# A chunk's scores on six levels of two sub-blocks instead of three levels of four, and unit 1's transposed keys copied by VectorE

## The reference

```python
for t in range(S):
    state = alpha[:, :, t, :, None] * state + np.einsum('bhd,bhe->bhde', k[:, :, t], v[:, :, t])
    y[:, :, t] = np.einsum('bhd,bhde->bhe', q[:, :, t], state)
x = y.transpose(0, 2, 1, 3).reshape(B * S, H * D)

p = domain_probs / (domain_probs.sum(-1, keepdims=True) + 1e-09)
for e in range(E):
    out += p[:, e:e + 1] * (np.maximum(x @ w1[e], 0.0) @ w2[e])

h = out @ w_in
result = (h - np.tanh(h)) @ w_out
```

## Time and profile before

| | us |
|---|---|
| median of 3 runs (lowest, highest) | 1383.19 (1381.79, 1383.29) |
| the profiled execution | 1381.91 |
| its span | 1380.1 |
| TensorE busy (share of the span) | 1338.2 (97%) |
| VectorE busy | 874.3 (63%) |
| ScalarE busy | 573.4 (42%) |
| GpSimd busy | 277.2 (20%) |
| mean granted clock of TensorE | 0.989 of full |

### The profile page before, as it was taken

How to read it: one execution, slowest core, us unless ns; L and a number is a source line. 1 busy time by engine, 2 the same in 40 slices (tenths; PEclk the granted TensorE clock), 3 DMA queues, 4 the chain that set the end, 5 groups by cost and what they waited for, 6 DMA issues and landing times.

```text
span 1380.1 us, 25841 instructions
## 1 busy us (share of the span) xinstructions
PE 1338.2 (97%) x10177; PEld 1121.9 (81%) x10177; DVE 874.3 (63%) x1767; ACT 573.4 (42%) x1072; POOL 277.2 (20%) x274
## 2 busy tenths in 40 slices
PE   3699999999999999999999999999999999999999
PEld 3578788988878888878898887888887889888888
DVE  8984855994654875465687565497556378323285
ACT  1525346843214751414662323374231476211175
POOL 4666654004022001313001403100221000000000
PEclk8799999999999999999999999999999999999999
DMA  7389797856655656565655655664665465655552
GB/s 217 92 306 321 240 323 242 322 212 219 211 196 197 231 181 218 181 211 196 242 183 179 222 194 199 207 229 169 216 211 172 161 220 189 222 185 200 180 193 89
DMA packets 104680, 289.08 MB, mean 209 GB/s; under 512 B 9936, under 2 KB 64432, under 8 KB 104560
## 3 DMA queue, kind: packets, MB, share of 16 engines
q1 hardware_dynamic: 104416, 287.23, 60.9%
q10 hardware_dynamic: 144, 0.20, 0.1%
HBM read 242.52 MB, written 42.52 MB: 207 GB/s over the span
## 4 chain that ended last, share of the span: by engine, by line
PE 89%; DVE 7%; ACT 2%; issue 1%; DMA 0%; DVEq 0%
PE bank L662 14%; PE bank L663 13%; PE bank L664 13%; PE bank L687 9%; PE bank L688 9%; PE bank L689 9%; PE bank L713 4%; PE bank L711 4%; PE bank L712 4%; PE bank L575 4%; PE bank L616 2%; PE bank L553 1%; DVE RG L1166 1%; PE bank L588 1%; DVE GG L1136 1%
## 5 line engine op out<-in xcount | busy, mean ns | idle before, releaser
L887 ACT ACTIVATE HH<-GG 128x512 fp32r<-128x512 f32 x192 | 121.2, 631 | 631.4 <-PE bank L689 509.2
L662 PE MATMUL bank<-XB,RG 128*128 128x512 f32 x864 | 348.5, 403 | 4.7 <-DVE GG L1109 2.2
L663 PE MATMUL bank<-XB,RG 128*128 128x512 f32 x864 | 339.4, 393 | 0.0
L664 PE MATMUL bank<-XB,RG 128*128 128x512 f32 x864 | 338.3, 392 | 0.0
L1109 DVE SCALAR_TENSOR_TENSOR GG<-bank,PB 128x512 f32<-128x512 f32 x192 | 133.4, 695 | 310.3 <-PE bank L664 310.0
L687 PE MATMUL bank<-HH,RG 128*128 128x512 f32 x576 | 224.3, 389 | 0.0
L688 PE MATMUL bank<-HH,RG 128*128 128x512 f32 x576 | 224.2, 389 | 0.0
L689 PE MATMUL bank<-HL,RG 128*128 128x512 f32 x576 | 224.0, 389 | 0.0
L1320 POOL TENSOR_TENSOR KU<-KU,TOT 128x256 f32<-128x256 f32 x88 | 68.5, 805 | 699.3 <-PE bank L575 699.3
L662 PEld LDWEIGHTS bank<-XB,RG 128*128 128x128 f32 x864 | 162.1, 188 | 45.9 <-issue 4.2
L664 PEld LDWEIGHTS bank<-XB,RG 128*128 128x128 f32 x864 | 162.2, 188 | 35.4
(11 more groups left out here) (129 smaller groups left out, 1676.8 us busy)
## 6 DMA issues: line engine op xcount, KB each, us to landing
RG<-scratch SPq DMA_DIRECT2D x240, 768.0 KB, 4.3
scratch<-RG SPq DMA_DIRECT2D x48, 768.0 KB, 5.3
VS<-vp SPq DMA_DIRECT2D x11, 768.0 KB, 6.0
WS<-w SPq DMA_DIRECT2D x32, 192.0 KB, 3.4
PB<-probs SPq DMA_DIRECT2D x6, 1024.0 KB, 7.0
AU<-qka SPq DMA_DIRECT2D x11, 512.0 KB, 5.3
R<-qka SPq DMA_DIRECT2D x11, 512.0 KB, 5.2
KU<-qka SPq DMA_DIRECT2D x11, 512.0 KB, 6.2
```

Source lines behind the costliest of these rows:

```text
L662: nc.tensor.matmul(out, w1(g, 0, kt), x_part(m, 0, kt), start=(kt == order[0]), stop=False)
L663: nc.tensor.matmul(out, w1(g, 0, kt), x_part(m, 1, kt), start=False, stop=False)
L664: last = nc.tensor.matmul(out, w1(g, 1, kt), x_part(m, 0, kt), start=False, stop=(kt == order[-1]))
L887: nc.scalar.activation(HH[:, h_slot(g)], GG[:, h_slot(g)], ACT.Copy).then_inc(high, 1)
```

## The change

The levels are now h = 1, 2, 4, 8, 16, 32, and each joins sub-blocks two by two. At a level only the queries of a pair's second sub-block meet the keys of its first: 32 moving columns for a chunk instead of 96. There are no distant slices any more; the queries stay in one tile QS, in place, and so does the rotation.

- `scores` has one part per level, 32 matmuls with 64 weight columns and 32 moving ones, at the steps `SCORES_AT` = 1, 2, 4, 5, 7, 8. A unit has 192 of these matmuls instead of 96.
- `rotate` is one product of 512 elements per partition at each level, `raise_keys` too. Both wait for the fills of their own level, and the next level waits for both. In a unit's slots VectorE rotates and picks, and GpSimd raises, at the same step as the scores.
- `pick` is two copies of 256 elements per level: 14 copies for a unit instead of 38, the diagonal's two among them.
- `tabulate` has six products instead of nine.
- In the start-up, unit 1's query product moves from GpSimd to VectorE, unit 1's keys are raised by VectorE at levels 1, 3 and 5 and its tables are made there too; unit 0's and unit 1's levels alternate on TensorE. The eight copies of unit 1's transposed keys (`lay(1, 0)`, `lay(1, 1)`) move from ScalarE to VectorE, and ScalarE's `join(0)` comes behind the copy of the transposed probabilities.

```diff
-LEVELS = [1, 4, 16]
+LEVELS = [1, 2, 4, 8, 16, 32]
+SCORES_AT = [1, 2, 4, 5, 7, 8]
-ROWS = 7
-QC = CH // 4 * ROWS
-SW = CH // 4 * (ROWS - 1)
-QL = UW // 4 * ROWS
+SW = CH // 2
+NL = len(LEVELS)
+PICKS = 2 * NL + 2
...
+        def halves(ap, h):
+
+            pairs = ap.rearrange("p (n two h) -> p n two h", two=2, h=h)
+            return pairs[:, :, 0, :], pairs[:, :, 1, :]
+
+        def queries(u):
+
+            return QS[2 if own(u) else turn_of(u) % 2]
...
-            def scores(u, level, half):
...
+            def scores(u, level):
+                if level == 0:
+                    pe.wait_ge(spread[own(u)], turn_of(u) + 1)
+                else:
+                    pe.wait_ge(keys_up[own(u)], NL * turn_of(u) + level)
+                    pe.wait_ge(rotated[own(u)], NL * turn_of(u) + level)
+                bank_free(u, 2 + 2 * level)
+                bank_free(u, 3 + 2 * level)
+                _, second = halves(queries(u)[:, :], LEVELS[level])
+                n = SW // LEVELS[level]
+                for m in range(2 * UC):
+                    for k in range(2):
+                        c = (m // UC * 2 + k) * UC + m % UC
+                        for o, keys, q in crossed(u, c, k):
+                            last = nc.tensor.matmul(fill_bank(u, 2 + 2 * level + k)[o, m * SW:m * SW + SW], keys,
+                                                    second[q, c * n:c * n + n, :], start=True, stop=True)
+                        if m == 2 * UC - 1:
                             last.then_inc(filled[own(u)], 1)
...
             lay(0, 0)
             lay(0, 1)
-            join(0)
-            lay(1, 0)
-            lay(1, 1)
             swap_totals(1)
             act.wait_ge(prob_turned, 1)
             nc.scalar.activation(PT[0:E * NTB * TT, :], bank[3][0:E * NTB * TT, 0:P], ACT.Copy).then_inc(prob_laid, 1)
+            join(0)
...
+            def pick(u, level):
                 h = LEVELS[level]
+                for k in range(2):
+                    dve.wait_ge(filled[own(u)], filled_at(u, 2 + 2 * level + k))
+                    dve.wait_ge(picked[own(u)], PICKS * turn_of(u) + 2 * level + k + 1)
...
+                    nc.vector.copy_predicated(dst, m.to_broadcast([P, 2, UC, SW // h, h]), src).then_inc(picked[own(u)], 1)
...
+                first, _, _ = tables(u, level)
+                dve.wait_ge(filled[own(u)], filled_at(u, 3 + 2 * level))
+                if level:
+                    dve.wait_ge(tabled[own(u)], NL * turn_of(u) + level)
+                _, q = halves(queries(u)[:, :], LEVELS[level])
+                nc.vector.tensor_tensor(q, q, first.to_broadcast([P, SPAN[level] // 2, LEVELS[level]]),
+                                        ALU.mult).then_inc(rotated[own(u)], 1)
...
-                    rotate(u, 0)
-                if step in (1, 2):
-                    pick(u, 0, step - 1)
...
+                if step in SCORES_AT:
+                    rotate(u, SCORES_AT.index(step))
+                    pick(u, SCORES_AT.index(step))
...
+            pick(0, 0)
+            for level in range(1, NL):
+                rotate(0, level)
+                tabulate(1, level, level + 1)
+                pick(1, level - 1)
+                rotate(1, level)
+                if level % 2:
+                    raise_keys(1, level)
+                pick(0, level)
+            pick(1, NL - 1)
             probabilities()
+            lay(1, 0)
+            lay(1, 1)
             states(0)
...
-                if step in (3, 6, 9):
-                    raise_keys(u, step // 3 - 1)
+                if step in SCORES_AT:
+                    raise_keys(u, SCORES_AT.index(step))
```

More of the change, by code:

```diff
@@ L62, with mask_at @@
 REST = C0 - C1 * C1 / (4 * C2)
[L65 to L66 removed]
+def mask_at(level):
+    return level * SW
 def level_masks():
@@ L289, in total @@
                 return T64[u % 2][:, :]
[L290 to L302, removed]
+            at = sum(SPAN[1:level])
+            return TOT[own(u)][:, at:at + SPAN[level]]
         def fill_bank(u, k):
@@ L556, in diagonal @@
                             last.then_inc(filled[own(u)], 1)
-            def scores(u, level, half):
[L559 to L572, removed]
-                        c = (2 * half + n) * UC + m
-                        for o, keys, q in crossed(u, c, n):
-                            last = nc.tensor.matmul(fill_bank(u, k + n)[o, m * SW:m * SW + SW], keys,
-                                                    rows[q, c * groups:c * groups + groups, h:ROWS * h],
-                                                    start=True, stop=True)
-                        if m == UC - 1:
+            def scores(u, level):
[15 more added lines that the diff above has]
+                        if m == 2 * UC - 1:
                             last.then_inc(filled[own(u)], 1)
@@ L1274, in _, with tabulate @@
         def _(pool):
-            def tabulate(u, first=0, last=9):
-                n = 9 * turn_of(u)
-                for i in range(first, last):
-                    t, two, three = tables(u, i // 3)
-                    if i:
-                        pool.wait_ge(tabled[own(u)], n + i)
-                    if i % 3 == 0:
-                        out, a, b = two, t[:, :, 0:3], t[:, :, 1:4]
-                    elif i % 3 == 1:
-                        out, a, b = three, two[:, :, 0:2], t[:, :, 2:4]
-                    else:
-                        out, a, b = total(u, i // 3 + 1).rearrange("p (n a) -> p n a", a=1), three[:, :, 0:1], t[:, :, 3:4]
-                    nc.gpsimd.tensor_tensor(out, a, b, ALU.mult).then_inc(tabled[own(u)], 1)
+            def tabulate(u, first=0, last=NL):
+                n = NL * turn_of(u)
+                for level in range(first, last):
+                    one, two, both = tables(u, level)
+                    if level:
+                        pool.wait_ge(tabled[own(u)], n + level)
+                    nc.gpsimd.tensor_tensor(both, one, two, ALU.mult).then_inc(tabled[own(u)], 1)
             def spread_queries(u):
```

289 lines of the change are left out of this document (88 added, 201 removed).

## The result

| | before | after |
|---|---|---|
| median of 4 runs each, us | 1382.5 (1380.2 to 1383.3) | 1391.4 (1390.0 to 1394.3) |
| ratio, 95% interval | | 1.007 (1.0048 to 1.0091) |
| profiled execution, us (span) | 1381.9 (1380.1) | 1390.0 (1388.2) |

The change makes the kernel 9 us slower. Forecast were 1397.3 us with a range of 1385 to 1406: the direction and the range hold, the size is 5.9 us too high.

A forecast was written before the change was run, and what follows sets the result against it. After about 67 us of start-up decided by chains across engines, TensorE's queue bounds the kernel. 1381.9 + 16.2 (score levels) - 4 (start-up) + 4 (unit 2) - 0.8 (later units) = 1397.3 us, range 1385 to 1406.

The forecast's parts named there:

- Later levels: Score products of the ten later units on TensorE: 60 levels dearer, +16.2 us, bounds -16.2 and +16.2.
- the term of 0.27 a level: Score products of later units: a level takes 1.09 us, the diagonal's time with the same weights, for 0.82 before.
- Rival 1: Score levels: moving columns bind, loads hide behind other quarters' matmuls, a level falls to 0.55 us; 1365 us, chance 0.09.
- rival 4: Score levels: a floor of 25.6 ns per matmul makes a level 1.64 us; 1430 us, chance 0.02.
- The lower bound in the argument: Score levels: a 64-column weight load takes about 0.055 us, so fewer moving columns cannot bring a quarter's records closer.
- Start-up: Units 0 and 1 before the first main product: unit 1's join ends earlier, -4 us, bounds -9 and 0.
- The text's own chain: End of the start-up: probabilities, TensorE's turning, then ScalarE's work; unit 1's join ends at 55.8 us instead of 60.4.
- the collision: Start-up levels: VectorE's rotation waits about 1.3 us for GpSimd's raising, making a pair of levels 4.5 us.
- Unit 2's second level: Start of the main stage: TensorE idles 6 us for raised keys behind GpSimd's splits, then half clock; +4 us, bounds 0 and +7.
- Later units: After unit 2: work between adjacent levels just fits, 0; a 0.83 us wait behind unit 3's rotation goes, -0.8 us.
- Rival 3: Later units: adjacent levels wait for a late VectorE, 30 x 0.5 = +15 us; 1412 us, chance 0.12.
- Rival 2: Start-up gains more (-9 us) and unit 2 hardly waits (0); 1388 us, chance 0.15.

The follow-up runs named there:

- the first two experiments: Changed kernel, score matmuls of units 2 to 11: first with 16 moving columns instead of 32, 1390.4 us; then with 32 weight columns instead of 64, 1370.5 us.
- the narrow weights: Changed kernel with the weights of levels 3 to 6 cut to 60, 56, 48 and 32 of 64 columns: 1383.2 us.

## Why the prediction was right, and where its sizes were off

**Later levels, +16.2 forecast, 60 x 0.22 = +13.2 measured.** The mechanism holds and was shown: the weight loads bind. Mis-sized was the term of 0.27 a level, taken from the diagonal. A level with 32 columns takes 1.06, not 1.09, which gives 0.24; over 47 levels the net is 0.22. The 0.03 between diagonal and level lie at the start of the group: the second round of four starts 107 ns behind the first in the diagonal and 79 in the level, and after that both take 58 ns a round. The 0.02 lie in the products behind a level, 4.31 us (386.49 to 390.80) for 4.35 before (386.89 to 391.24); why they are shorter is not shown. Rival 1 (columns) and rival 4 (a floor) fell with the first two experiments, and the decision between them could be read ahead from the rows, as it was: the diagonal against the step with 96 columns. The lower bound in the argument, two weight loads 0.11 us apart, was the right thing to look at. The Trainium skill (TensorE: Matmul & The Clock Gate, "LDWEIGHTS (loading the stationary operand)") says that a load's time goes with its columns and not its rows, 1/1.2 ns each. The trace agrees: 16 columns fewer in each quarter's 16 loads would be 0.213 us by it, and 64 to 48 columns took 0.21 off. From 48 to 32 it was 0.16, where single gaps of up to 49 ns stand between rounds 32 ns apart. The 64 columns of 16 loads would be 0.85 us by that rule, an estimate, so about 0.2 us of a level's 1.06 is something else.

**Start-up, -4 forecast, -6.3 measured.** The step's path was right: the last scores were copied at 41.65 us where the text had 42, and ScalarE's chain decides from there. The text's own chain gave 60.4 - 55.8 = 4.6 us and was written as 4 without a reason. Unit 1's join ended at 54.76 for 55.8, mostly because the probabilities took 1.4 us and not 2.7; GpSimd no longer works beside them (its next row begins as they end). From the end of that join to the first main product it then took 5.9 us for 6.6, where the text had no change; that part was not traced. So the product came at 60.64, not near 63.

A pair of levels took VectorE 4.3 us (five from 20.31 to 41.65) for 4.5, but two errors cancel in this. The two copies of a level took 0.67 us from start to start at h of 4 and more, as forecast, but 1.1 at h = 1 and 2; the row that the price came from, at 25.87, is a level with h = 4. And the collision cost less.

The collision is there, but uneven: rotations took 1.14 and 1.27 us at 29.37 and 33.09, and 0.68 alone. VectorE's timeline, then GpSimd's:

```profile
33.09 1.27 DVE L959 TENSOR_TENSOR QS<-QS,TOT 128x512 f32<-128x512 f32 x1
...
36.90 0.69 DVE L959 TENSOR_TENSOR QS<-QS,TOT 128x512 f32<-128x512 f32 x1 [0.34 <-PE bank L553]
```

```profile
32.74 1.07 POOL L1222 TENSOR_TENSOR KU<-KU,TOT 128x512 f32<-128x512 f32 x1 [2.79 <-PE bank L553]
...
36.95 1.56 POOL L1222 TENSOR_TENSOR KU<-KU,TOT 128x512 f32<-128x512 f32 x1
```

Where the raising had started first, the rotation took longer; where the rotation started first, by 0.05 us, the raising did. Of the twelve rotations in this profile four were lengthened (0.88 to 1.27 us), four started 0.04 or 0.05 us ahead of their raising, and four had no raising beside them. Had every rotation stood behind its raising, there would have been no gain. Reordering VectorE's queue only moved the meetings.

**Unit 2's second level, +4 forecast, +2.2 measured** (2.65 less two levels' 0.22). The chain named is the one in the trace, and moving the raising removed it. The text had the level 14.0 us behind the first main product; it was 12.2. Each link was a little shorter: SP's last issue for slot 7 came 5.0 us behind that product for 5.5, its high part was split at 8.4 for 9.8, GpSimd's split ended at 10.7 for 11.6, and the raising took 1.5 us, not 2.3. Half clock followed the wait, as said. TensorE waited 4.49 us there where the text had about 6.

**Later units.** -0.8 for unit 3's wait came true. Rival 3 did not: no level of the later units waits. Rival 2, at 1388, came nearer to the measured 1391.4 than the forecast did, and half of it happened: the start-up gained 6.3 of its 9 us, but unit 2 did wait.

In sum 13.2 - 6.3 + 2.2 - 0.8 = +8.3, against 8.1 between the spans. The three mis-sized terms were 3.0, 2.3 and 1.8 us too dear. They err the same way, so none hid another, and against the profiled execution (1390.0) the forecast is 7.3 us too high. The range of 21 us was wide enough to hold that.

## What to carry to other kernels

Splitting an engine's products into more and smaller ones, to spare another engine, is not free: a product with 64 weight columns and 64 or fewer moving ones here costs its weight load, so twice as many matmuls of a third of the columns were dearer, though they stream a third less. Look for weight columns that no result uses before cutting moving ones. And where a change adds a dependence to an engine off the path, read that engine's queue at the place: moving one raise ahead of two splits was worth 3.6 us on top of the narrow weights.

## What the runs showed of the hardware that was not expected

- *Granted clock in the start-up.* The changed kernel's levels at 20 to 40 us ran at 0.50 in one profile and at 1.00 in another, with TensorE busy 18.5 and 18.0 of 20 us. Where they ran at 1.00, the first main products were in part at half clock; the two executions ended 1.4 us apart, the one with the full-clock start-up later. It is not a trade of one for the other: with the key copies back on ScalarE both stretches were slow, 0.50 at 20 to 40 us and 0.86 at 60 to 72.
- *Masked copies by run length.* VectorE's pair of copies of 256 elements from PSUM took 1.29 us at h = 1 (22.55), 1.31 at h = 2 (24.87) and 0.76 at h of 4 and more (28.70), though element counts are equal. GpSimd was idle beside the first and busy beside the other two.
- *VectorE beside GpSimd.* The 512-element product of two SBUF tensors took 2.05 us for 0.69 when it started 0.04 us behind a GpSimd product of 1.54 us: it ended 0.55 us behind that product, so this is GpSimd's time and then its own, not a shared pace. The Trainium skill (SBUF — State Buffer, "SBUF: two separate sides") calls it an exclusive lock, and this row agrees, as do the rows at 32.74 to 36.95 above, with the engine that starts first unharmed.
- *The wait that hides the clock.* Half clock in the first main products put unit 2's first level 1.8 us later and its second only 0.7, where GpSimd's raising decided.
